# A radix search for a routing threshold on one Trainium2 core: the digit found is handed to all partitions by a matmul instead of by a transposing reduction

## The chip, the cores and the metric

One core of a Trainium2 chip runs the whole program. The metric is device time in microseconds (us), the median of three runs. Engines are named as in the profile: PE is TensorE (PEld its weight loads), DVE VectorE, ACT ScalarE, POOL GpSimd, SP the queue that issues DMAs.

## The reference

The computation is a chain of three layers. A decayed linear attention over 4 batches, 8 heads, 768 steps and head size 64 gives 3072 rows of 512. A greedy mixture of experts follows: each of 8 experts takes at most 384 tokens, in the order of the logits. A gated unit ends it.

```python
def _moe_ref(x, w_gate, w1, w2):
    cap = N // E                        # 384
    logits = x @ w_gate
    for idx in np.argsort(-logits.flatten()):
        tok, e = idx // E, idx % E
        if assigned[tok] >= 0 or counts[e] >= cap: continue
        assigned[tok] = e; counts[e] += 1
    for e in range(E):
        out[assigned == e] = np.maximum(x[assigned == e] @ w1[e], 0) @ w2[e]

def _moe2_ref(x, w_gate, w_val, w_out):
    return (sigmoid(x @ w_gate) * (x @ w_val)) @ w_out
```

## The kernel before

**Attention block (lines 268 to 663).** 24 units (4 batches, 6 chunks of 128 steps) pass through a software pipeline on all engines. `scale_k` (L454, POOL) makes the tile `ks` that PE transposes one slot later (L600). Between the second and the third `scale_k` POOL also makes the constant tables of the routing (`number_tables`, `filled_tables`), between the third and the fourth the tables derived from others (`derived_tables`); `link` lets POOL wait for each such instruction before the next.

**Routing.** Rather than sort, the kernel closes one expert at a time. One routing finds the threshold key at which some expert fills up, marks the tokens above it as assigned, numbers the members of the expert that is full, and gathers their rows. A key has 32 bits, taken as `DIGITS` = 7 digits of 5 bits, `RADIX` = 32. Per digit there were two visits of PE:

- DVE compares all keys with the 32 rungs of `ladder` (`compare`, L861, two halves into `above`); PE counts per expert and rung (L1129, 6 matmuls); DVE copies the counts (L911, `partial`);
- PE folds them (L1138, 4 matmuls into `PS_K`); DVE runs `threshold` (L871 compare with `room`, L872 maximum, giving one `flag` per partition, L873 a transposing reduction that adds the flags of each group of 32 partitions and leaves the sum on all of them, `digit_at`); then DVE makes the next key (L916, `prefix`) and compares again, and `raise_by` (L867) prepares the digit after that.

After the digits come the visits `V_TIE` (L1142 to L1144), `V_COUNT` (L1146), `V_RANK` (L1149, L1150) and `V_IDS` (L1155).

**Rounds.** The first routing stands alone, with nothing beside it. Then come 8 rounds of `one_round`. A round computes one expert and the gated unit for its 384 tokens with three matmuls per product (high and low parts, L1168 to L1170 with 384 columns, L1246 to L1248 with 512). In the first seven rounds the routing of the next expert is threaded between these matmuls. Where a visit stands on PE is set by the table `visit_at`: `step` counts the columns that PE has streamed, 2200 of them are one planned us (`us(t)`), and after each group of three matmuls the visits that are due are issued. PE runs in order and has no other way round a visit whose data isn't there. On DVE, whose queue is in order too, `route_until` puts the DVE part of a visit ahead of the next `h_low`, `h2_low` or `product` once the planned time has passed; `piece_low` (L1028) makes low parts of streamed weights, and `p_low` (L1023) the low part of the product `pf` (L1019).

In each digit of the plan, 6.8 planned us long, the counting visit stood at 0 and the folding visit at 2.2. The round loop is a hardware loop on DVE, ACT, POOL and SP for rounds 0 to 6, and unrolled on PE. In round 0 alone, POOL still makes low parts of resident weights (L262) as its `gate_done` and `val_done` come.

Of the kernel before, what the change touches and what calls it, by code (L numbers as in the profile page):

```python
# [13 lines left out]
P = 128  # L14


def retention_moe_glu_kernel(nc, q, k, v, w_router, w1, w2, w_gate, w_val, w_out, decay, out):
# [14 lines left out]
    with ctx:  # L32
        def sb(name, shape, dt):
            return ctx.enter_context(nc.sbuf_tensor(name, shape, dt))
# [17 lines left out]
        DIGITS = -(-32 // RADIX_BITS)  # L52
        NEG = -3.4028234663852886e38
        BIG = 1.0e6
        PREP_CHAIN = 13
        ROUTE_CHAIN = 78
        CHAIN_START = PREP_CHAIN
        TABLES = 7 + (TT - 1) + 6 + 3 + 3

        RING = 8  # L60
        STREAMED = KF + 2 * KD + RING
# [9 lines left out]
        V_TIE = 2 * DIGITS  # L71
        FOLD = P // RADIX
        V_COUNT = V_TIE + 1
        V_RANK = V_COUNT + 1
# [22 lines left out]
        def us(t):  # L97
            return int(t * COLUMNS_PER_US)

        DIGIT_GAP, LATE_GAP, PART_GAP = us(6.8), us(5), us(2)  # L100
        visit_at = [us(1) + vis // 2 * DIGIT_GAP + us((0, 2.2)[vis % 2]) for vis in range(2 * DIGITS)]
        visit_at += [visit_at[-1] + (n + 1) * LATE_GAP for n in range(3)]
        expert_at = visit_at[V_RANK]
        part_at = [expert_at + us(1) + n * PART_GAP for n in range(PARTS)]
# [42 lines left out]
        counted_fresh = sb("counted_fresh", [P, E], BF16)  # L147
        partial = sb("partial", [P, E, FOLD], F16)
        reached = sb("reached", [P, E], BF16)
        flag = sb("flag", [P, 1], F32)  # L150
        digit_at = sb("digit_at", [P, 1], F32)
        expert_f = sb("expert_f", [P, 1], F32)
        expert_id = sb("expert_id", [P, 1], I32)
        id_sums = sb("id_sums", [P, TT + 1], F32)
# [3 lines left out]

        segment = sb("segment", [P, E, U], BF16)
        unit_ones = sb("unit_ones", [P, U], BF16)  # L160
        ladder = sb("ladder", [P, RADIX], F32)
        raised = sb("raised", [P, U], F32)
# [5 lines left out]
        edges = sb("edges", [P, TT - 1], F32)  # L168
        below = sb("below", [P, P], BF16)
        ones = sb("ones", [P, P], BF16)  # L170
        fold = sb("fold", [P, FOLD, FOLD, RADIX], F16)
        at_above = nc.sbuf_base
        above = sb("above", [P, U, RADIX], BF16)
# [94 lines left out]
        with ExitStack() as actx:  # L268
# [113 lines left out]
            def _(pool):  # L382
# [17 lines left out]
                def number_tables():  # L400
                    count(column[:, :], [[1, P]], 0)
                    count(expert_iota[:, :], [[1, E]], 0)
                    count(priority[:, :], [[-1, E]], E)
                    count(position[:, :, 0], [[0, U]], 0, 1)
                    count(position[:, :, 1], [[P, U]], 0)
                    count(ladder[:, :], [[1, RADIX]], 1)
                    count(shift[:, :], [[-RADIX_BITS, DIGITS]], RADIX_BITS * (DIGITS - 1))

                def filled_tables():
                    for j in range(TT - 1):  # L410
                        fill(edges[:, j:j + 1], float((j + 1) * P))
                    fill(ones[:, :], 1.0)
                    fill(fold[:, :, :, :], 0.0)
                    fill(below[:, :], 1.0)
                    fill(segment[:, :, :], 1.0)
                    fill(unit_ones[:, :], 1.0)
                    fill(id_sums[:, TT:TT + 1], 0.0)
                    fill(unassigned[:, :], 1.0)
                    fill(assigned[:, :, :], 0.0)
                    fill(room[:, :], float(CAP))  # L420

                def derived_tables():
                    pool.wait_ge(tables_made, made[0])
                    link(nc.gpsimd.memset(segment[:, :, 0:1], 0.0))

                    link(pool.affine_select(out=below[:, :], in_=below[:, :], compare_op=ALU.is_gt, fill=0.0,
                                            base=0, pattern=[[1, P]], channel_multiplier=-1))
                    link(pool.affine_select(out=fold[:, :, :, :], in_=fold[:, :, :, :], compare_op=ALU.not_equal, fill=1.0,
                                            base=0, pattern=[[-RADIX, FOLD], [0, FOLD], [-1, RADIX]], channel_multiplier=1))
                    assert made[0] == TABLES, made[0]  # L430
# [400 lines left out]
        def _(dve):  # L831
# [22 lines left out]
            def flat(ap):  # L854
                return ap.rearrange("p e u -> p (e u)")

            def compare(keys):

                for half in range(2):
                    tiles = slice(half * U // 2, (half + 1) * U // 2)  # L860
                    nc.vector.tensor_tensor(above[:, tiles, :], keys[:, tiles].unsqueeze(2).to_broadcast([P, U // 2, RADIX]),  # L861
                                            ladder[:, :].unsqueeze(1).to_broadcast([P, U // 2, RADIX]),
                                            ALU.is_ge).then_inc(route_ready if half else half_compared, 1)

            def raise_by(keys, j):

                count_only(nc.vector.scalar_tensor_tensor(raised[:, :], keys, float(RADIX), digit_f[:, j, :], ALU.mult, ALU.add))  # L867
# [35 lines left out]
            def route(vis, i):  # L903

# [1 line left out]
                    return  # L906

                dve.wait_ge(route_done, i * VISITS + vis)
                if vis < V_TIE and vis % 2 == 1:

                    nc.vector.tensor_copy(partial[:, :, :], PS_R[:, 0:FOLD * E].rearrange("p (e t) -> p e t", e=E)).then_inc(route_ready, 1)  # L911
                elif vis < V_TIE:

                    j = vis // 2
                    threshold()
                    link(nc.vector.scalar_tensor_tensor(prefix[:, :], digit_at[:, :].to_broadcast([P, U]), -float(RADIX),  # L916
                                                        raised[:, :], ALU.mult, ALU.add))
                    compare(prefix)
                    if j + 1 < DIGITS:
                        raise_by(prefix[:, :], j + 1)  # L920
                elif vis == V_TIE:

                    threshold()
                    count_only(nc.vector.tensor_scalar(is_on[:, :], prefix[:, :], digit_at[:, :], None, ALU.is_equal))
                    link(nc.vector.tensor_scalar(is_above[:, :], prefix[:, :], digit_at[:, :], None, ALU.is_gt))
# [192 lines left out]
        def _(pe):  # L1118
            pe.wait_ge(tables_made, TABLES)

            def visit(vis, i):
                if vis < V_TIE and vis % 2 == 0:

                    for t in range(0, U, FOLD):
                        if t == 0:
                            pe.wait_ge(half_compared, i * DIGITS + vis // 2 + 1)
# [8 lines left out]
                if vis < V_TIE:  # L1135
# [178 lines left out]
```

## Time and profile before

| | |
|---|---|
| median of 3 runs | 1115.22 us (1115.11 to 1117.47) |
| the profiled execution | 1115.11 us, of which the span of instructions is 1113.0 us |
| PE busy | 1050.6 us, 94% of the span |
| DVE busy | 632.1 us, 57% |
| ACT busy | 344.3 us, 31% |
| POOL busy | 132.6 us, 12% |
| PE's share of the chain that ended last | 81% |

The profile shows one execution. The span runs from its first to its last instruction; the 2.1 us to the execution's own time lie around it. Matmuls are pipelined, so that a matmul's duration overlaps the next one's; what a matmul costs in a stream is read from the distance of the starts. Idle time is given ahead of a row in square brackets, with what ended it.

### The profile page before, as it was taken

How to read it: one execution, taken by the hardware profiler on the slowest of the kernel's cores; microseconds unless marked ns; L12 is line 12 of the kernel's file. 1: busy time of each engine (PE TensorE's matmuls, PEld its weight loads, DVE VectorE, ACT ScalarE, POOL GpSimd, SP SyncE). 2: the span in 40 equal slices, each digit the busy share in tenths (PEclk: the TensorE clock that was granted, in tenths of full speed). 3: DMA queues.
4: the chain of work that ended last, by engine and by line, in shares of the span. 5: the costliest groups of instructions: out<-in, count | busy, mean ns of one | idle time of the engine just before them, and what ended most of it. 6: DMA issues, size and time to landing. Idle time of an engine off the chain costs nothing.

```text
span 1113.0 us, 20477 instructions
## 1 busy us (share of the span) xinstructions
PE 1050.6 (94%) x7536; PEld 973.7 (87%) x7536; DVE 632.1 (57%) x1720; ACT 344.3 (31%) x659; POOL 132.6 (12%) x159
## 2 busy tenths in 40 slices
PE   6999922999999999999999999999999999999996
PEld 5888812989999999999999999999999999999995
DVE  3665468778366646664566456654675476634211
ACT  3444422332243224322432234223422342224210
POOL 5555301033010101000100110011001100110001
PEclk9999955999999999999999999999999999999998
DMA  9999443312041213212321222122312131214000
GB/s 205 246 243 246 111 125 104 115 39 85 20 124 58 69 37 105 77 48 57 98 83 48 58 86 95 39 67 71 110 39 67 58 115 38 67 54 118 18 1 28
DMA packets 172988, 96.69 MB, mean 87 GB/s; under 512 B 80224, under 2 KB 158048, under 8 KB 172896
## 3 DMA queue, kind: packets, MB, share of 16 engines
q1 hardware_dynamic: 169056, 82.92, 28.1%
q0 software_dynamic: 3840, 12.59, 3.8%
q8 instruction: 52, 0.85, 0.3%
q14 instruction: 40, 0.33, 0.1%
HBM read 82.90 MB, written 12.58 MB: 86 GB/s over the span
## 4 chain that ended last, share of the span: by engine, by line
PE 81%; DVE 4%; issue 1%; POOL 0%; DMA 0%; ACT 0%; DVEq 0%; POOLq 0%
PE bank L1168 21%; PE bank L1170 20%; PE bank L1169 20%; PE bank L1246 6%; PE bank L1248 6%; PE bank L1247 6%; PE bank L1163 1%; PE bank L1129 1%; DVE above L861 1%; PE bank L1138 1%; PE bank L1155 0%; DVE onehot L977 0%; DMA xg<-xrows,ids 0%; DVE ring L1028 0%; POOL out_dram L743 0%
## 5 line engine op out<-in xcount | busy, mean ns | idle before, releaser
L1168 PE MATMUL bank<-h2h,resident 128*128 128x384 f32 x768 | 260.7, 339 | 0.0
L1170 PE MATMUL bank<-h2h,resident 128*128 128x384 f32 x768 | 257.9, 336 | 0.0
L1169 PE MATMUL bank<-h2l,resident 128*128 128x384 f32 x768 | 257.4, 335 | 0.0
L1019 DVE TENSOR_TENSOR pf<-bank,gate 128x384 f32<-128x384 f32 x96 | 53.4, 556 | 167.3 <-PE bank L1170 167.1
L1169 PEld LDWEIGHTS bank<-h2l,resident 128*128 128x128 f32 x768 | 144.2, 188 | 3.4
L1168 PEld LDWEIGHTS bank<-h2h,resident 128*128 128x128 f32 x768 | 144.2, 188 | 3.5
L1170 PEld LDWEIGHTS bank<-h2h,resident 128*128 128x128 f32 x768 | 144.1, 188 | 0.0
L773 ACT ACTIVATE ring<-ring_raw 128x512 fp32r<-128x512 f32 x192 | 118.3, 624 | 64.5 <-DMA ring_raw<-in_moe_w_out_dram 41.9
L1028 DVE TENSOR_TENSOR ring<-ring_raw,ring 128x512 fp32r<-128x512 f32 x192 | 127.4, 689 | 0.0
L793 ACT ACTIVATE ph<-pf 128x384 fp32r<-128x384 f32 x96 | 50.4, 525 | 240.8 <-DVE pf L1019 240.8
L789 ACT ACTIVATE gate<-bank 128x384 f32<-128x384 f32 x96 | 47.1, 491 | 201.2 <-PE bank L1170 198.5
L1168 PE MATMUL bank<-xh,ring 128*128 128x384 f32 x256 | 89.1, 348 | 0.0
L1168 PE MATMUL bank<-hh,ring 128*128 128x384 f32 x256 | 88.7, 346 | 0.0
L1023 DVE TENSOR_TENSOR pl<-pf,ph 128x384 fp32r<-128x384 f32 x96 | 54.7, 570 | 56.8 <-ACT ph L793 56.8
L1170 PE MATMUL bank<-xh,ring 128*128 128x384 f32 x256 | 85.9, 336 | 0.0
L1169 PE MATMUL bank<-xl,ring 128*128 128x384 f32 x256 | 85.8, 335 | 0.0
L1170 PE MATMUL bank<-hh,ring 128*128 128x384 f32 x256 | 85.8, 335 | 0.0
L1169 PE MATMUL bank<-hl,ring 128*128 128x384 f32 x256 | 85.7, 335 | 0.0
L729 POOL DMA_INDIRECT xg<-xrows,ids x24 | 23.7, 986 | 499.4 <-DVE ids L993 494.5
L1246 PE MATMUL bank<-ring,ph 128*128 128x512 f32 x192 | 76.6, 399 | 0.0
L1248 PE MATMUL bank<-ring,pl 128*128 128x512 f32 x192 | 75.8, 395 | 0.0
L1247 PE MATMUL bank<-ring,ph 128*128 128x512 f32 x192 | 75.6, 394 | 0.0
(170 smaller groups left out, 1671.6 us busy)
## 6 DMA issues: line engine op xcount, KB each, us to landing
ring_raw<-in_moe_w_dram SPq DMA_DIRECT2D x128, 256.0 KB, 3.0
ring_raw<-in_moe_w_out_dram SPq DMA_DIRECT2D x64, 256.0 KB, 2.9
qraw<-in_q_dram SPq DMA_DIRECT2D x24, 256.0 KB, 4.5
kraw<-in_k_dram SPq DMA_DIRECT2D x24, 256.0 KB, 5.1
vraw<-in_v_dram SPq DMA_DIRECT2D x24, 256.0 KB, 5.2
xrows<-xrow SPq DMA_DIRECT2D x24, 256.0 KB, 4.0
resident_raw<-in_moe_w_gate_dram SPq DMA_DIRECT2D x12, 256.0 KB, 4.5
resident_raw<-in_moe_w_val_dram SPq DMA_DIRECT2D x12, 256.0 KB, 4.7
```

Source lines behind the costliest of these rows:

```text
L773: nc.scalar.activation(ring[:, n % RING, 0, :], ring_raw[n % RING][:, :], ACT.Copy).then_inc(piece_hi, 1)
L789: nc.scalar.activation(gate[:, f % 2, :], bank[2 * (f % 2)][:, 0:CAP], ACT.Sigmoid).then_inc(gate_ready, 1)
L793: nc.scalar.activation(ph[:, f % 2, :], pf[:, f % 2, :], ACT.Copy).then_inc(ph_ready, 1)
L1019: nc.vector.tensor_tensor(pf[:, f % 2, :], bank[2 * (f % 2) + 1][:, 0:CAP], gate[:, f % 2, :], ALU.mult).then_inc(p_ready, 1)
L1023: nc.vector.tensor_tensor(pl[:, f % 2, :], pf[:, f % 2, :], ph[:, f % 2, :].bitcast(F32), ALU.subtract).then_inc(pl_ready, 1)
L1028: nc.vector.tensor_tensor(ring[:, s, 1, :], ring_raw[s][:, :], ring[:, s, 0, :].bitcast(F32), ALU.subtract).then_inc(piece_lo, 1)
L1168: nc.tensor.matmul(ps, wh, xhi, start=start, stop=False)
L1169: nc.tensor.matmul(ps, wh, xlo, start=False, stop=False)
L1170: return nc.tensor.matmul(ps, wl, xhi, start=False, stop=stop)
L1246: nc.tensor.matmul(PS_OUT[j][:, :], ph[:, f % 2, toks], wh, start=f == 0, stop=False)
L1247: nc.tensor.matmul(PS_OUT[j][:, :], ph[:, f % 2, toks], wl, start=False, stop=False)
L1248: last = nc.tensor.matmul(PS_OUT[j][:, :], pl[:, f % 2, toks], wh, start=False, stop=f == KG - 1)
```

## The change

Per digit there are now three visits. DVE stops after the maximum (`flag`, now bf16) and signals PE. PE multiplies the flags of all 128 partitions by a constant matrix `weighted_ones[:, j, :]`, whose entries are 32^-j / 4; the sum, times that weight, stands in `PS_K[:, 0:1]` on every partition. DVE reads it from there as a per-partition scalar. The digits are weighted in advance (`digit_f` times 32^-j) and each digit has its own ladder, so that keys need no raising; `raise_by` goes. The added tables are made by POOL: `weight` and `weighted_ones` in `filled_tables`, six ladders in `derived_tables`. The plan keeps 6.8 planned us per digit, with visits at 0, 1.7 and 4; the visits after the digits follow 1.8 planned us later than before.

```diff
-        visit_at = [us(1) + vis // 2 * DIGIT_GAP + us((0, 2.2)[vis % 2]) for vis in range(2 * DIGITS)]
+        visit_at = [us(1) + vis // 3 * DIGIT_GAP + us((0, 1.7, 4)[vis % 3]) for vis in range(3 * DIGITS)]
...
-        flag = sb("flag", [P, 1], F32)
-        digit_at = sb("digit_at", [P, 1], F32)
+        flag = sb("flag", [P, 1], BF16)
...
                 def filled_tables():
+                    for j in range(DIGITS):
+                        fill(weight[:, j:j + 1], float(RADIX) ** -j)
+                        fill(weighted_ones[:, j, :], float(RADIX) ** -j / FOLD)
...
                 def derived_tables():
                     pool.wait_ge(tables_made, made[0])
+                    for j in range(1, DIGITS):
+                        link(nc.gpsimd.tensor_scalar(ladder[:, j, :], ladder[:, 0, :], float(RADIX) ** -j, None, ALU.mult))
...
-            def threshold():
-
-                link(nc.vector.tensor_tensor(reached[:, :], PS_K[:, 0:E], room[:, :], ALU.is_ge))
-                link(nc.vector.reduce_max(flag[:, :], reached[:, :], AX_X))
-                link(nc.vector.tensor_reduce(digit_at[:, :], flag[:, :].to_broadcast([P, RADIX]), axis=AX_X, op=ALU.add,
-                                             apply_transpose=True))
...
-                link(nc.vector.tensor_scalar(digit_f[:, :, :], digit_i[:, :, :], 1.0, None, ALU.add))
-                compare(digit_f[:, 0, :])
-                raise_by(digit_f[:, 0, :], 1)
+                link(nc.vector.scalar_tensor_tensor(digit_f[:, :, :], digit_i[:, :, :], 1.0,
+                                                    weight[:, :].unsqueeze(2).to_broadcast([P, DIGITS, U]), ALU.add, ALU.mult))
+                compare(0, digit_f[:, 0, :])
...
+                elif vis < V_TIE and vis % 3 == 2:
+
+                    link(nc.vector.tensor_tensor(reached[:, :], PS_K[:, 0:E], room[:, :], ALU.is_ge))
+                    nc.vector.reduce_max(flag[:, :], reached[:, :], AX_X).then_inc(route_ready, 1)
                 elif vis < V_TIE:
 
-                    j = vis // 2
-                    threshold()
-                    link(nc.vector.scalar_tensor_tensor(prefix[:, :], digit_at[:, :].to_broadcast([P, U]), -float(RADIX),
-                                                        raised[:, :], ALU.mult, ALU.add))
-                    compare(prefix)
-                    if j + 1 < DIGITS:
-                        raise_by(prefix[:, :], j + 1)
+                    j = vis // 3
+                    link(nc.vector.scalar_tensor_tensor(prefix[:, :], digit_f[:, 0, :] if j == 1 else prefix[:, :], PS_K[:, 0:1],
+                                                        digit_f[:, j, :], ALU.subtract, ALU.add))
+                    compare(j, prefix)
...
+                elif vis < V_TIE:
+
+                    last = nc.tensor.matmul(PS_K[:, 0:1], weighted_ones[:, vis // 3, :], flag[:, :], start=True, stop=True)
```

On PE, in a round, four groups of three matmuls behind the folding visit of a digit (`hh` and `ring` are the operands of the expert's second product), before:

```order
L1169 MATMUL bank<-hl,ring 128x384
L1170 MATMUL bank<-hh,ring 128x384
L1168 MATMUL bank<-hh,ring 128x384
L1169 MATMUL bank<-hl,ring 128x384
L1170 MATMUL bank<-hh,ring 128x384
```

The same place in the changed kernel, whose lines are numbered 3 lower here:

```order
L1166 MATMUL bank<-hl,ring 128x384
L1167 MATMUL bank<-hh,ring 128x384
L1136 MATMUL bank<-flag,weighted_ones 128x1
L1165 MATMUL bank<-hh,ring 128x384
L1166 MATMUL bank<-hl,ring 128x384
```

One matmul with one moving column is added between two groups, once per digit.

On DVE, in a round, at the start of the gated unit (`pf` and `pl` belong to its first tile; `ring_raw_82` and `ring_raw_83` are streamed pieces), before:

```order
L838 REGISTER_ALU
L916 SCALAR_TENSOR_TENSOR prefix<-digit_at,raised 128x24
L838 REGISTER_ALU
L861 TENSOR_TENSOR above<-prefix,ladder 128x384 x2
L1019 TENSOR_TENSOR pf<-bank,gate 128x384
L1023 TENSOR_TENSOR pl<-pf,ph 128x384
L1027 REGISTER_ALU
L1028 TENSOR_TENSOR ring<-ring_raw_82,ring 128x512
L1027 REGISTER_ALU
L1028 TENSOR_TENSOR ring<-ring_raw_83,ring 128x512
L908 REGISTER_ALU
L911 CAST partial<-bank 128x32
```

And in the changed kernel:

```order
L1013 TENSOR_TENSOR pf<-bank,gate 128x384
L1017 TENSOR_TENSOR pl<-pf,ph 128x384
L1021 REGISTER_ALU
L1022 TENSOR_TENSOR ring<-ring_raw_82,ring 128x512
L1021 REGISTER_ALU
L1022 TENSOR_TENSOR ring<-ring_raw_83,ring 128x512
L902 REGISTER_ALU
L913 SCALAR_TENSOR_TENSOR prefix<-prefix,bank,digit_f 128x24
L843 REGISTER_ALU
L866 TENSOR_TENSOR above<-prefix,ladder 128x384 x2
L902 REGISTER_ALU
L905 CAST partial<-bank 128x32
```

The last comparison of the routing moves from ahead of the product `pf` to behind both pieces.

On POOL, in the attention block, from the last filled tables to the fourth `scale_k`, before:

```order
L398 MEMSET room 128x8
L454 TENSOR_TENSOR ks<-kraw,dec 128x512
L424 MEMSET segment 128x8
L426 AFFINE_SELECT below<-below 128x128
L428 AFFINE_SELECT fold<-fold 128x512
L454 TENSOR_TENSOR ks<-kraw,dec 128x512 x4
```

And in the changed kernel:

```order
L398 MEMSET room 128x8
L459 TENSOR_TENSOR ks<-kraw,dec 128x512
L428 TENSOR_SCALAR ladder<-ladder 128x32 x6
L429 MEMSET segment 128x8
L431 AFFINE_SELECT below<-below 128x128
L433 AFFINE_SELECT fold<-fold 128x512
L459 TENSOR_TENSOR ks<-kraw,dec 128x512 x4
```

Six instructions, each waited for, come ahead of the fourth `ks`. Fourteen `MEMSET` rows, seven of 128x1 and seven of 128x128, come ahead of the third.

## Rows read from the trace of the kernel before

**Rows 1.** Busy time (us, share, instructions), and granted clock in 40 slices
```profile
PE 1050.6 (94%) x7536; PEld 973.7 (87%) x7536; DVE 632.1 (57%) x1720; ACT 344.3 (31%) x659; POOL 132.6 (12%) x159
...
PEclk9999955999999999999999999999999999999998
```

**Rows 2.** PE's waits, 195 to 1113: for whom, us in total, times, longest
```profile
PE bank L1142 <- DVE tied_before L932: 1.1, 1, 1.1
```

**Rows 3.** Timeline of PE around L1146: start, duration, line, shapes
```profile
365.39 0.33 PE L1169 MATMUL bank<-h2l,resident 128*128 128x384 f32 x1
365.57 0.34 PE L1170 MATMUL bank<-h2h,resident 128*128 128x384 f32 x1
365.75 0.18 PE L1146 MATMUL bank<-counted_fresh,ones 128*128 128x8 bf16 x1
365.79 0.48 PE L1246 MATMUL bank<-ring,ph 128*128 128x512 f32 x1
366.10 0.39 PE L1247 MATMUL bank<-ring,ph 128*128 128x512 f32 x1
366.33 0.40 PE L1248 MATMUL bank<-ring,pl 128*128 128x512 f32 x1
```

**Rows 4.** Timeline of PE around a counting visit of six matmuls
```profile
345.09 0.34 PE L1170 MATMUL bank<-h2h,resident 128*128 128x384 f32 x1
345.27 0.32 PE L1129 MATMUL bank<-choice,above 128*128 128x32 bf16 x6
345.43 0.42 PE L1168 MATMUL bank<-h2h,resident 128*128 128x384 f32 x1
345.69 0.33 PE L1169 MATMUL bank<-h2l,resident 128*128 128x384 f32 x1
```

**Rows 5.** Timeline of POOL, 2 to 19
```profile
2.28 1.20 POOL L444 TENSOR_SCALAR_AFFINE_SELECT pick<-pick 128x8 f32<-128x8 f32 x4
...
13.36 0.20 POOL L398 MEMSET ones<- 128x128 bf16 x1
13.50 0.52 POOL L398 MEMSET fold<- 128x512 f16 x1
...
14.37 0.09 POOL L398 MEMSET id_sums<- 128x1 f32 x1
14.40 0.11 POOL L398 MEMSET unassigned<- 128x24 f32 x1
...
18.30 1.48 POOL L454 TENSOR_TENSOR ks<-kraw,dec 128x512 f32<-128x512 f32 x1 [0.81 <-DMA vraw<-in_v_dram]
```

**Rows 6.** Timeline of PE, 16 to 20
```profile
16.23 0.66 PE L600 MATMUL bank<-ident,ks 128*128 128x128 f32 x4 [0.20 <-POOL ks L454]
...
19.89 0.61 PE L600 MATMUL bank<-ident,ks 128*128 128x128 f32 x4
```

**Rows 7.** PE's busy time in stretches: us, PE busy first, granted clock
```profile
17.00:30.00 13.00, 13.00 (x218) 11.80 (x216) 7.10 (x14) 5.80 (x12) 5.07 (x4) 1.00 1.22 245
30.00:60.00 30.00, 29.70 (x447) 26.19 (x446) 19.66 (x33) 13.52 (x29) 15.32 (x14) 1.00 1.01 241
60.00:90.00 30.00, 30.00 (x459) 26.77 (x455) 18.78 (x35) 13.08 (x28) 15.37 (x15) 1.00 1.05 243
```

**Rows 8.** Timeline of one digit of the first routing, and of L1144
```profile
150.60 0.16 DVE L872 TENSOR_REDUCE flag<-reached 128x1 f32<-128x8 bf16 x1
150.79 0.21 DVE L873 TRANSPOSE_TENSOR_REDUCE digit_at<-flag 128x1 f32<-128x32 f32 x1
151.04 0.18 DVE L916 SCALAR_TENSOR_TENSOR prefix<-digit_at,raised 128x24 f32<-128x24 f32 x1
151.26 1.03 DVE L861 TENSOR_TENSOR above<-prefix,ladder 128x384 bf16<-128x384 f32 x2
...
170.46 0.21 PE L1144 MATMUL bank<-counted,ones 128*128 128x8 bf16 x1
170.71 0.16 DVE L935 TENSOR_TENSOR limit<-room,bank 128x8 f32<-128x8 f32 x1 [0.60 <-PE bank L1144]
```

**Rows 9.** Timeline of DVE at the start of round 1
```profile
307.50 1.88 DVE L1034 COPY orow<-bank 128x512 f32<-128x512 f32 x3
311.22 0.19 DVE L911 CAST partial<-bank 128x32 f16<-128x32 f32 x1 [1.84 <-issue]
```

**Rows 10.** Timeline of DVE in round 1, from the first product
```profile
350.25 0.55 DVE L1019 TENSOR_TENSOR pf<-bank,gate 128x384 f32<-128x384 f32 x1
351.39 0.56 DVE L1023 TENSOR_TENSOR pl<-pf,ph 128x384 fp32r<-128x384 f32 x1 [0.59 <-ACT ph L793]
351.87 1.29 DVE L1028 TENSOR_TENSOR ring<-ring_raw,ring 128x512 fp32r<-128x512 f32 x2
353.07 0.18 DVE L911 CAST partial<-bank 128x32 f16<-128x32 f32 x1
```

**Rows 11.** Timeline of DVE and POOL in round 0
```profile
236.64 2.38 DVE L1028 TENSOR_TENSOR ring<-ring_raw,ring 128x512 fp32r<-128x512 f32 x2
...
237.08 1.39 POOL L262 TENSOR_TENSOR resident<-resident_raw,resident 128x512 fp32r<-128x512 f32 x1 [0.79 <-PE bank L1170]
```

More of the change, by code:

```diff
@@ L54, in retention_moe_glu_kernel @@
         BIG = 1.0e6
-        PREP_CHAIN = 13
-        ROUTE_CHAIN = 78
+        PREP_CHAIN = 12
+        ROUTE_CHAIN = 58
         CHAIN_START = PREP_CHAIN
-        TABLES = 7 + (TT - 1) + 6 + 3 + 3
+        TABLES = 7 + 3 * DIGITS - 1 + (TT - 1) + 6 + 3 + 3
         RING = 8
@@ L69, in retention_moe_glu_kernel @@
         assert KF == RING and 2 * KD == RING and OUT_STREAMED <= KG and TT == 3 and LATE % LATE_EACH == 0
-        V_TIE = 2 * DIGITS
+        V_TIE = 3 * DIGITS
         FOLD = P // RADIX
@@ L160, in retention_moe_glu_kernel @@
         unit_ones = sb("unit_ones", [P, U], BF16)
-        ladder = sb("ladder", [P, RADIX], F32)
-        raised = sb("raised", [P, U], F32)
+        ladder = sb("ladder", [P, DIGITS, RADIX], F32)
+        weight = sb("weight", [P, DIGITS], F32)
         shift = sb("shift", [P, DIGITS], I32)
@@ L170, in retention_moe_glu_kernel @@
         ones = sb("ones", [P, P], BF16)
+        weighted_ones = sb("weighted_ones", [P, DIGITS, P], BF16)
         fold = sb("fold", [P, FOLD, FOLD, RADIX], F16)
@@ L405, in number_tables @@
                     count(position[:, :, 1], [[P, U]], 0)
-                    count(ladder[:, :], [[1, RADIX]], 1)
+                    count(ladder[:, 0, :], [[1, RADIX]], 1)
                     count(shift[:, :], [[-RADIX_BITS, DIGITS]], RADIX_BITS * (DIGITS - 1))
                 def filled_tables():
+                    for j in range(DIGITS):
+                        fill(weight[:, j:j + 1], float(RADIX) ** -j)
+                        fill(weighted_ones[:, j, :], float(RADIX) ** -j / FOLD)
                     for j in range(TT - 1):
@@ L855, in flat, with compare @@
                 return ap.rearrange("p e u -> p (e u)")
-            def compare(keys):
+            def compare(j, keys):
                 for half in range(2):
@@ L861, in compare @@
                     nc.vector.tensor_tensor(above[:, tiles, :], keys[:, tiles].unsqueeze(2).to_broadcast([P, U // 2, RADIX]),
-                                            ladder[:, :].unsqueeze(1).to_broadcast([P, U // 2, RADIX]),
+                                            ladder[:, j, :].unsqueeze(1).to_broadcast([P, U // 2, RADIX]),
                                             ALU.is_ge).then_inc(route_ready if half else half_compared, 1)
-            def raise_by(keys, j):
-                count_only(nc.vector.scalar_tensor_tensor(raised[:, :], keys, float(RADIX), digit_f[:, j, :], ALU.mult, ALU.add))
-            def threshold():
-                link(nc.vector.tensor_tensor(reached[:, :], PS_K[:, 0:E], room[:, :], ALU.is_ge))
-                link(nc.vector.reduce_max(flag[:, :], reached[:, :], AX_X))
-                link(nc.vector.tensor_reduce(digit_at[:, :], flag[:, :].to_broadcast([P, RADIX]), axis=AX_X, op=ALU.add,
-                                             apply_transpose=True))
             def prepare():
@@ L908, in route @@
                 dve.wait_ge(route_done, i * VISITS + vis)
-                if vis < V_TIE and vis % 2 == 1:
+                if vis < V_TIE and vis % 3 == 1:
                     nc.vector.tensor_copy(partial[:, :, :], PS_R[:, 0:FOLD * E].rearrange("p (e t) -> p e t", e=E)).then_inc(route_ready, 1)
+                elif vis < V_TIE and vis % 3 == 2:
+                    link(nc.vector.tensor_tensor(reached[:, :], PS_K[:, 0:E], room[:, :], ALU.is_ge))
+                    nc.vector.reduce_max(flag[:, :], reached[:, :], AX_X).then_inc(route_ready, 1)
                 elif vis < V_TIE:
-                    j = vis // 2
-                    threshold()
-                    link(nc.vector.scalar_tensor_tensor(prefix[:, :], digit_at[:, :].to_broadcast([P, U]), -float(RADIX),
-                                                        raised[:, :], ALU.mult, ALU.add))
-                    compare(prefix)
-                    if j + 1 < DIGITS:
-                        raise_by(prefix[:, :], j + 1)
+                    j = vis // 3
+                    link(nc.vector.scalar_tensor_tensor(prefix[:, :], digit_f[:, 0, :] if j == 1 else prefix[:, :], PS_K[:, 0:1],
+                                                        digit_f[:, j, :], ALU.subtract, ALU.add))
+                    compare(j, prefix)
                 elif vis == V_TIE:
-                    threshold()
-                    count_only(nc.vector.tensor_scalar(is_on[:, :], prefix[:, :], digit_at[:, :], None, ALU.is_equal))
-                    link(nc.vector.tensor_scalar(is_above[:, :], prefix[:, :], digit_at[:, :], None, ALU.is_gt))
+                    count_only(nc.vector.tensor_scalar(is_on[:, :], prefix[:, :], PS_K[:, 0:1], None, ALU.is_equal))
+                    link(nc.vector.tensor_scalar(is_above[:, :], prefix[:, :], PS_K[:, 0:1], None, ALU.is_gt))
                     link(nc.vector.tensor_tensor(tied[:, :, :], choice[:, :, :], per_token(is_on[:, :]), ALU.mult))
@@ L1121, in visit @@
             def visit(vis, i):
-                if vis < V_TIE and vis % 2 == 0:
+                if vis < V_TIE and vis % 3 == 0:
                     for t in range(0, U, FOLD):
                         if t == 0:
-                            pe.wait_ge(half_compared, i * DIGITS + vis // 2 + 1)
+                            pe.wait_ge(half_compared, i * DIGITS + vis // 3 + 1)
                         if t == U // 2:
@@ L1134, in visit @@
                     pe.wait_ge(route_ready, i * (VISITS - 1) + vis + 1)
-                if vis < V_TIE:
+                if vis < V_TIE and vis % 3 == 1:
                     for t in range(FOLD):
```

## The prediction

> **What bounds the kernel now.** I read the busy times first: PE has 94% of the span, the next engine 57% [rows 1]. Then PE's waits in the rounds, from 195 on: in 918 us PE waits once, 1.1 us, for DVE at a `V_TIE` visit; that is in round 0 [rows 2]. So in the rounds PE is the bound, and what DVE needs for a digit costs nothing as long as it is ready when PE comes. A change there is worth what it adds to PE's stream, and whatever wait it makes. Then the stretches of the attention block: PE is busy without a gap from 17 on, at the full granted clock of 2.4 GHz [rows 7]; there too a delay of PE is never made good. Only the first routing, about 145 to 183, is a chain of DVE and PE with nothing beside it, in the slices whose granted clock is 0.5, that is 1.2 GHz [rows 1].
>
> **The rounds: 49 more visits.** Seven rounds with a routing, seven digits each, one more matmul. No row shows a matmul of one column, but L1146 is a visit of one matmul with 8 columns and the same kind of stationary matrix. Undisturbed matmuls of 384 columns start 0.17 to 0.18 apart (365.39, 365.57) and those of 512 columns 0.23 apart (366.10, 366.33) [rows 3]. From 365.57 to 366.10 would then be 0.18 for L1170 and 0.23 for L1246, 0.41; it is 0.53. The visit costs 0.12. A counting visit of six matmuls: from 345.09 to 345.69 is 0.60, of which two matmuls of 384 would take 0.35, so 0.25 [rows 4]. Between one and six matmuls the cost rises by 0.13, about 0.026 a matmul, and 0.10 stands for the visit as such: PE stops for the semaphore and can't load weights ahead. I take 0.13 for each new visit, since nearly all stand between matmuls of 384 columns: 49 x 0.13 = 6.4. Bounds: 0.026, if only the step per matmul were paid, gives 1.3; 0.15 gives 7.4.
>
> The Trainium skill ("TensorE: Matmul & The Clock Gate", section "Wait — 56ns, not 53.3ns?") says that start to start never drops below about 25 ns, however few columns a matmul has. The 0.026 per matmul inside a visit agrees with it. Taken as the whole price of one more small matmul it would make an estimate of 49 x 0.025 = 1.2; the 0.12 of the lone visit speaks against that.
>
> **New waits of PE in the rounds.** I went through a round of the plan, placing each visit at its group of three matmuls (0.52 a group) and each DVE part behind what stands ahead of it. Four places are near.
>
> - *The first fold of a round.* At the loop's turn DVE idles 1.84 after the rows' copies and makes `partial` at 311.22 to 311.41 [rows 9]. The fold was due five groups behind the counting visit (3.2 planned us), now four (2.7): with the count at 309.04, four groups 2.08 and 0.25 for the visit, at 311.37. From `partial`'s end to a matmul's start there are some 0.06, so PE waits 0.1, in six rounds 0.6. In round 0 DVE comes to it late by its eight pieces; I count 0.3 more. Together 0.9, bounds 0 and 2.
> - *The last counting visit.* Its comparison now stands behind `pf`, `pl` and two pieces, where it stood ahead of them. I count from the start of the counting visit before it, which is at 345.27 [rows 4]. PE: 0.25 for that visit, four groups, 0.2 for the fold, four groups, 0.13 for the new visit, five groups: 13 x 0.52 + 0.58 = 7.3. DVE: the gated unit's first tile ends one group behind the fold, and the product can start at 3.3, as it no longer waits for the comparison; `pl` starts 1.14 later, the pieces 0.48 after that, and `prefix`, where `partial` stood, 1.20 later, at 6.1 [rows 10]. With 0.28 for `prefix` and 1.03 for both halves the first is ready at 6.95, the second at 7.43. PE comes at 7.3, and 0.1 later wants the second: the first is in time, the second some 0.07 late with its signal: 7 x 0.07 = 0.5. Bounds 0, and 7 if the slip is 1 in each round.
> - *The same in round 0.* There a DVE operation that comes while POOL works on resident weights starts only as POOL ends: two pieces took 2.38 instead of 1.29 beside L262 [rows 10, 11]. In the new order the second piece meets POOL's instruction before that one, and the comparison comes about 1.0 to 1.4 late. I take 1.0, bounds 0 and 1.5.
> - *`V_TIE` in round 0.* Between the last fold and this visit, 5.0 planned us, DVE had a product, a piece, the threshold and the visit's own work to do, and came 1.1 late [rows 2]. Now product, piece and threshold lie ahead of the new visit, and only the visit's own work lies in the 5.0 behind it. The wait goes: -1.1. Bounds -1.1 and 0.
>
> The Trainium skill ("SBUF — State Buffer", section "SBUF: two separate sides") says that a DVE instruction with two SBUF inputs contends with a GpSimd instruction that reads SBUF, and that the loser blocks for the whole instruction. The trace agrees: 1.09 more for two pieces beside one of 1.39. By it the round-0 wait is a full one rather than shared.
>
> All other DVE parts are ready 0.2 to 1.8 before PE comes; the nearest is the fourth digit's `partial`, behind `h2l` and two pieces, 0.2 early. Later visits move 1.8 planned us back; `ids` are wanted only 30 us later.
>
> **The tables.** POOL makes 14 more fills ahead of the third `ks`. A fill of 128x128 bf16 takes 0.14 (13.36 to 13.50), one of 128x1 0.03 (14.37 to 14.40) [rows 5]: 7 x 0.17 = 1.2. PE already waits for this `ks`, 0.20 at 16.23 [rows 6], so nothing covers it: 1.2 on the path. Then six linked multiplications come ahead of the fourth `ks`. Nearest rows: the linked `pick`, four in 1.20, so 0.3 each, 1.8 in all [rows 5]. Of 1.2 + 1.8 = 3.0, POOL's idle 0.81 at 18.30 is cover; that `ks` starts at 20.5 and ends, 1.48 later, at 22.0. PE wants it at 19.89 + 1.2 = 21.1 [rows 6]: 0.9 more. Sum 2.1. PE makes none of it good up to the end of the block [rows 7]. Bounds: 1.2 if the multiplications are hidden, 3.0 if each takes 0.45; 0 only if a later wait took it up, and there is none.
>
> **The first routing.** From `flag` to `prefix` lie 0.44 now (150.60, 151.04), with L873 between [rows 8]. New: `flag` 0.16, some 0.06 to PE, a matmul to the instruction behind it 0.25, as L1144 to L935 (170.46, 170.71): 0.47. So 0.03 for each of 7 digits, 0.2. `prefix` now takes a scalar per partition from PSUM; no row has that form, I take 0.06 more, 6 x 0.06 = 0.4. The L867 that goes stood in the shadow of PE's counting. `digit_f` with a second input: 0.1. Sum 0.7. Bounds: -0.7 (0.1 less per digit) and 1.8 (0.25 more).
>
> **Sum.** 6.4 + 0.9 + 0.5 + 1.0 - 1.1 + 2.1 + 0.7 = 10.5. The profiled execution took 1115.11 with a span of 1113.0; 1115.1 + 10.5 = 1125.6. That execution is 0.1 from the median of 1115.22. I forecast 1125.5.
>
> **Rivals.**
>
> - *Lone matmuls are cheap.* A one-column matmul may cost PE only the 0.026 of a further matmul in a visit: 1.3 instead of 6.4, so 10.5 - 5.1 = 5.4, 1120.5. For it: within a visit the price is that low [rows 3, 4]. Against it: L1146 is alone as well, and costs 0.12. 8%.
> - *A wait in each round.* If `prefix` and both halves come 1 us later at the last counting visit, or `partial` of the fourth digit does at its fold, each round pays a wait of 0.8: 7 x 0.8 = 5.6 more, 1131. For it: 0.2 and less of slack at both. Against: in round 1 the pieces take 1.29, in the regular step [rows 10]. 12%.
> - *The tables are hidden*, by a faster POOL or a later wait: 8.4, 1123.5. It lies in the main case's range; 10% of its own.
> - *Faster.* PE's chain per digit is shorter by a transposing reduction and L867 on DVE. If the new visits fell into PE's own shadow and the tables too, `V_TIE` would give 1.1 and the first routing 0.7: 1115.1 - 1.8 = 1113.3. What decides is the visit's price: up to 1.8 / 49 = 0.04 each it is no slower. Against: PE has no idle time in the rounds that could hold a visit [rows 2]. 3%.
>
> The forecast has the remaining 67%. Its own range is 1123.5 to 1128. Down to the cheap matmuls and up to part of the waits, the range for 8 in 10 is 1121 to 1130. About 0.2%, 2.2 us, is what can be told from no change; the last rival's 3% lie mostly within that: faster by more than it 1%, within it 3%, slower 96%.
>
> **What would show it.** PE's row of the new matmul with 56 in the profile, 49 of them in the rounds, each adding 0.12 to 0.14 between its neighbours' starts; a round in PE's repeated rows longer by 1.0 to 1.1; POOL named as what PE waits for at the third and fourth `ks`, about 1.4 and 0.9; the first routing's digit 0.1 longer; no `V_TIE` wait. Wrong it would be if PE waited more than 0.5 for DVE in each round, if the new visit cost under 0.05, or if the attention block ended at the same time as before.

## The result, and the profile after

The changed kernel takes 1127.53 us (median of 4 runs, 1126.45 to 1129.05), the kernel before, run beside it, 1115.54. The ratio is 1.0105, with a 95% interval from 1.0092 to 1.0118: it is slower, by about 12 us. The profiled execution took 1127.42 with a span of 1125.7. The forecast was 1125.5 with 1121 to 1130.

The busy times of the page, which answer to [rows 1]:

```profile
PE 1061.6 (94%) x7592; PEld 974.9 (87%) x7592; DVE 614.2 (55%) x1615; ACT 345.2 (31%) x659; POOL 133.7 (12%) x179
```

DVE has 105 instructions and 18 us less, and it buys nothing: PE has 56 instructions and 11 us more, still 94% of the span. To see where the time went, I cut the span at PE's transposes of the gathered rows, since each round begins with twelve of them. The view of that tile on PE gives the first and the last start; the kernel before, and then the one after:

```profile
L1163 PE MATMUL bank<-ident,xg x96: 272/273/475, 189.5 to 992.4; 128*128 128x128 f32 x96
```
```profile
L1160 PE MATMUL bank<-ident,xg x96: 270/272/474, 192.1 to 1005.0; 128*128 128x128 f32 x96
```

The first start is 2.6 later, the last one 12.6 later; behind it nothing changes. Read with each round's first transpose from PE's timeline, the 12.7 of the span are:

| part | before | after | more | forecast |
|---|---|---|---|---|
| start to the first routing | 144.82 | 146.83 | 2.0 | 2.1 |
| first routing, gather | 44.73 | 45.29 | 0.6 | 0.7 |
| round 0 | 115.03 | 119.19 | 4.2 | 1.2 |
| rounds 1 to 6 together | 6 x 114.44 | 692.54 | 5.9 | 6.5 |
| last part | 121.8 | 121.8 | 0.0 | 0 |

(Forecast by part: in round 0, seven lone matmuls 0.9, fold 0.3, last count 0.1, the same beside POOL 1.0, `V_TIE` -1.1; in the six others 5.5, 0.6 and 0.4.)

**The new visit.** PE's timeline around one of the new matmuls, as in [rows 3]:

```profile
349.69 0.33 PE L1166 MATMUL bank<-hl,ring 128*128 128x384 f32 x1
349.86 0.34 PE L1167 MATMUL bank<-hh,ring 128*128 128x384 f32 x1
350.04 0.18 PE L1136 MATMUL bank<-flag,weighted_ones 128*128 128x1 bf16 x1
350.08 0.42 PE L1165 MATMUL bank<-hh,ring 128*128 128x384 f32 x1
350.34 0.34 PE L1166 MATMUL bank<-hl,ring 128*128 128x384 f32 x1
```

From 349.86 to 350.34 is 0.48; two matmuls of 384 columns would take 0.35. The visit costs 0.13, though its own row is followed by the next start after only 0.04. The loss shows in the next two starts (0.04 + 0.26), so it can be read only over several rows. Over all 49 such visits the mean is 0.132.

**Round 0.** PE's waits from 195 on, which answer to [rows 2]:

```profile
PE bank L1123 <- DVE above L866: 1.8, 2, 1.3
```

The wait at `V_TIE` is gone, and two at the last counting visit have come. DVE, POOL and PE there, from their three timelines:

```profile
239.81 1.26 DVE L913 SCALAR_TENSOR_TENSOR prefix<-prefix,bank,digit_f 128x24 f32<-128x24 f32 x1
241.11 2.09 DVE L866 TENSOR_TENSOR above<-prefix,ladder 128x384 bf16<-128x384 f32 x2
```
```profile
239.19 1.85 POOL L262 TENSOR_TENSOR resident<-resident_raw,resident 128x512 fp32r<-128x512 f32 x1 [0.92 <-PE bank L1167]
241.27 1.52 POOL L262 TENSOR_TENSOR resident<-resident_raw,resident 128x512 fp32r<-128x512 f32 x1 [0.23 <-PE bank L1167]
```
```profile
241.72 0.24 PE L1123 MATMUL bank<-choice,above 128*128 128x32 bf16 x3 [0.54 <-DVE above L866]
243.26 0.24 PE L1123 MATMUL bank<-choice,above 128*128 128x32 bf16 x3 [1.30 <-DVE above L866]
...
245.07 0.63 PE L1243 MATMUL bank<-ring,ph 128*128 128x512 f32 x1
245.50 0.63 PE L1244 MATMUL bank<-ring,ph 128*128 128x512 f32 x1
```

`prefix`, undisturbed 0.24 to 0.25, lasts 1.26 and ends with POOL's first operation (239.19 + 1.85 = 241.04, against 241.07). The first half of `above` starts ahead of POOL's second operation and keeps its 0.56; the second half lasts 1.62 where e6 below has 0.55, and ends at 243.20, 0.41 behind that operation (241.27 + 1.52 = 242.79). PE waits 0.54 and 1.30. Then a thing that the forecast did not have: matmuls of 512 columns start 0.43 apart instead of 0.23 [rows 3]. PE's busy time in stretches of one execution, granted clock behind it, says why:

```profile
236.00:240.00 4.00, 4.00 (x28) 1.00 0.00 0
240.00:244.00 4.00, 2.17 (x16) 1.00 0.00 0
244.00:248.00 4.00, 4.00 (x17) 0.57 0.00 0
```

PE stood 1.8 of 4 us, and in the 4 us behind that the clock was 0.57 on average (2.4 GHz to start with, then 1.2, then 2.4 again): 4 x 0.43 = 1.7 us lost. The page's 40 slices show nothing of it.

**The tables.** POOL's timeline, as in [rows 5], and PE's, as in [rows 6]:

```profile
13.31 0.09 POOL L398 MEMSET weight<- 128x1 f32 x1
13.35 0.19 POOL L398 MEMSET weighted_ones<- 128x128 bf16 x1
...
14.54 0.12 POOL L398 MEMSET edges<- 128x1 f32 x2
...
15.96 1.04 POOL L459 TENSOR_TENSOR ks<-kraw,dec 128x512 f32<-128x512 f32 x1
17.08 2.58 POOL L428 TENSOR_SCALAR ladder<-ladder 128x32 f32<-128x32 f32 x6
...
21.18 2.49 POOL L459 TENSOR_TENSOR ks<-kraw,dec 128x512 f32<-128x512 f32 x2
```
```profile
17.05 0.66 PE L605 MATMUL bank<-ident,ks 128*128 128x128 f32 x4 [0.64 <-POOL ks L459]
...
22.28 0.66 PE L605 MATMUL bank<-ident,ks 128*128 128x128 f32 x4 [1.41 <-POOL ks L459]
```

The fourteen fills take 1.23. The six multiplications take 2.58, 0.43 each, where 0.3 was assumed. PE takes up the fourth `ks` at 22.28, 2.4 later than the 19.89 of before. At the end of the block 2.0 of the 2.4 are left.

**The first routing**, DVE's and PE's timelines of a digit, as in [rows 8]:

```profile
152.69 0.16 DVE L909 TENSOR_REDUCE flag<-reached 128x1 bf16<-128x8 bf16 x1
153.13 0.25 DVE L913 SCALAR_TENSOR_TENSOR prefix<-digit_f,bank 128x24 f32<-128x24 f32 x1 [0.28 <-PE bank L1136]
153.41 1.03 DVE L866 TENSOR_TENSOR above<-prefix,ladder 128x384 bf16<-128x384 f32 x2
```
```profile
152.91 0.18 PE L1136 MATMUL bank<-flag,weighted_ones 128*128 128x1 bf16 x1 [0.46 <-DVE flag L909]
```

From `flag` to `prefix` it is 0.44, as before: the way over PE costs what the transposing reduction did. `prefix` takes 0.25 instead of 0.18, and that is the difference, 0.07 a digit.

### The profile page after: what moved, and what is told of

The parts are those of the page before. It is cut to its first block, busy times and chain, and to the rows that moved or that the text cites. A ratio compares the mean times of both kernels' runs of the same rounds, so it can differ in the third digit from the quotient of the medians.

```text
span 1125.7 us, 20462 instructions
## 1 busy us (share of the span) xinstructions
PE 1061.6 (94%) x7592; PEld 974.9 (87%) x7592; DVE 614.2 (55%) x1615; ACT 345.2 (31%) x659; POOL 133.7 (12%) x179
## 4 chain that ended last, share of the span: by engine, by line
PE 82%; DVE 3%; issue 1%; POOL 0%; DMA 0%; ACT 0%; DVEq 0%; POOLq 0%
PE bank L1165 21%; PE bank L1167 20%; PE bank L1166 20%; PE bank L1243 6%; PE bank L1245 6%; PE bank L1244 6%; PE bank L1160 1%; PE bank L1123 1%; DVE above L866 1%; PE bank L1132 1%; PE bank L1152 0%; DVE onehot L971 0%; DMA xg<-xrows,ids 0%; DVE prefix L913 0%; POOL out_dram L748 0%
## 5 line engine op out<-in xcount | busy, mean ns | idle before, releaser
L1017 DVE TENSOR_TENSOR pl<-pf,ph 128x384 fp32r<-128x384 f32 x96 | 53.7, 560 | 52.9 <-ACT ph L798 52.7
```

Source lines behind the costliest of these rows:

```text
L1017: nc.vector.tensor_tensor(pl[:, f % 2, :], pf[:, f % 2, :], ph[:, f % 2, :].bitcast(F32), ALU.subtract).then_inc(pl_ready, 1)
```

## The experiments

**What does one more small matmul cost PE, and why?** The forecast had put 0.10 of the 0.13 down to PE's stop for the semaphore. The rival was the matmul's position alone between large ones. The kernel before gets 49 matmuls of one column, seven in a round, once without a wait, once with one on a semaphore long since raised, and once ahead of the fold's four.

```
e1   + if into is not None and lone[0] < DIGITS and us(5.5) + lone[0] * DIGIT_GAP <= at[0]:
     +     nc.tensor.matmul(into[:, 400:401], ones[:, :], unit_ones[:, 0:1], start=False, stop=False)
     +     lone[0] += 1
e2   +     pe.wait_ge(tables_made, TABLES)          (ahead of the matmul)
e3   + if i > 0:                                    (in visit, ahead of the fold's loop)
     +     nc.tensor.matmul(PS_K[:, 200:201], ones[:, :], unit_ones[:, 0:1], start=True, stop=True)
```

> The kernel before, with one more matmul of one moving column, with no consumer and no wait of its own, between two groups of three matmuls, once per digit in each of seven rounds: 49 in all. Theory A (a small matmul alone between large ones costs PE 0.13, because the next large weight load has nothing to hide behind): a round is 7 x 0.13 = 0.9 longer, the whole 6.4 us. Theory B (what costs is the stop for the semaphore, 0.10 of the 0.13): without a wait each costs 0.03, a round is 0.2 longer, the whole 1.3 us.

> The same 49 matmuls at the same places, each behind a wait for a semaphore that was reached long before. Both theories expect 6.4 us, 0.9 a round; if this is dearer than the kernel without the waits, the difference is the wait's.

> The same 49 matmuls, each put at the head of the folding visit of its digit, so that visit has five small matmuls instead of four. Both theories expect the step per matmul inside a visit, 0.026 each: 1.3 us in all, 0.2 a round. If it is 6 us instead, a small matmul costs 0.13 wherever it stands.

Measured beside a before of 1116.61: e1 1122.83 (ratio 1.0055, 1.0039 to 1.0072), e2 1123.29 (1.0056, 1.0039 to 1.0073), e3 1119.49 (1.0024, 1.0014 to 1.0033). A round of 114.44 became 115.38 in both e1 and e2 (0.94, 0.134 for each matmul) and 114.79 in e3 (0.35, 0.050 each, where both theories had 0.2). PE's timeline in e1, then in e3:

```profile
330.53 0.34 PE L1170 MATMUL bank<-hh,ring 128*128 128x384 f32 x1
330.71 0.18 PE L1180 MATMUL bank<-unit_ones,ones 128*128 128x1 bf16 x1
330.75 0.42 PE L1168 MATMUL bank<-hh,ring 128*128 128x384 f32 x1
331.01 0.34 PE L1169 MATMUL bank<-hl,ring 128*128 128x384 f32 x1
```
```profile
335.59 0.34 PE L1172 MATMUL bank<-hh,ring 128*128 128x384 f32 x1
335.77 0.18 PE L1137 MATMUL bank<-unit_ones,ones 128*128 128x1 bf16 x1
335.81 0.24 PE L1140 MATMUL bank<-partial,fold 128*128 128x8 f16 x4
335.91 0.42 PE L1170 MATMUL bank<-hh,ring 128*128 128x384 f32 x1
336.17 0.34 PE L1171 MATMUL bank<-hl,ring 128*128 128x384 f32 x1
```

The starts around e1's matmul, which waits for nothing, are those of the changed kernel's visit to 0.01. So the semaphore is not the cause, and this sentence of the forecast falls; its price stands. What costs is that a small matmul stands by itself: in company it costs 0.05, twice the forecast's 0.026 for a further one. That the hidden part is the loading of the next large matmul's weights fits the late second start (0.26), but no run took that load away.

**Round 0.** The fall of the clock was expected to go if PE did not stand. Two edits of the changed kernel bring this about in different ways: e5 has the one-column matmul ahead of the last counting visit 1.0 planned us earlier (38.0 instead of 39.0), so that DVE's `prefix` comes before its pieces; e6 takes POOL's operations out of DVE's way.

```
e5   + visit_at[17] = us(38.0)
e6   - pool.wait_ge(val_done if k % 2 else gate_done, k // 2 + 1)
     + pool.wait_ge(val_done if k % 2 else gate_done, k // 2 + 3)
```

> The changed kernel with one number of the plan changed: the last digit-making matmul in a round stands at 38.0 planned us instead of 39.0, so that DVE's last comparison goes between the product and its low part, ahead of the two pieces. Theory W (in round 0 the comparison queues behind pieces that meet POOL's work, PE waits 1.8 for it, and the pause lets the clock fall to 1.2 GHz for some 3.5 us): both go in round 0, 1.8 + 1.7 = 3.5 us less, so 1124.0; the other rounds keep their length within 0.1. Rival: the clock falls for another reason; then only 1.8 us go.

> The changed kernel with POOL's twelve low parts of resident weights in round 0 waiting for tiles two further on, so that none of them is beside the last comparison; the plan is untouched. If POOL's instruction is what makes the comparison late (theory W), PE waits under 0.1 at the last counting visit in round 0 too, as in the other rounds, and 3.5 us go. If the order on DVE alone makes it late, the 1.8 stay.

Measured beside a before of 1116.4: e5 1124.07 (1.0067, 1.005 to 1.0083), e6 1124.27 (1.0068, 1.0051 to 1.0085). Round 0 fell from 119.19 to 115.28 and 115.37, and the stretches of PE in e6 have no low clock any more:

```profile
236.00:240.00 4.00, 4.00 (x28) 1.00 0.00 0
240.00:244.00 4.00, 4.00 (x29) 1.00 0.00 0
244.00:248.00 4.00, 4.00 (x25) 1.00 0.02 4
```

DVE's timeline in e6, at the place where `prefix` took 1.26 and `above` 2.09:

```profile
239.87 0.24 DVE L913 SCALAR_TENSOR_TENSOR prefix<-prefix,bank,digit_f 128x24 f32<-128x24 f32 x1
240.14 1.02 DVE L866 TENSOR_TENSOR above<-prefix,ladder 128x384 bf16<-128x384 f32 x2
```

Both remove 3.8 to 3.9, more than the waits of 1.84, and 1.84 + 1.7 = 3.5 of it are the waits and the clock. So PE's standing comes from DVE's operations beside POOL's. The Trainium skill ("SBUF — State Buffer", section "SBUF: two separate sides"), named in the forecast for the full wait, was borne out: `prefix` ended 0.03 behind POOL's operation, and the half of `above` that met the next one ended only behind it too.

The low clock is less sure than the waits. No execution without the two waits has it. With them, it came again when the changed kernel was profiled once more (e10): round 0 118.78, clock 0.50 from 243.7 to 247.1. But in e4, the changed kernel with later tables (below), PE waited the same twice and the clock stayed:

```profile
242.24 0.24 PE L1123 MATMUL bank<-choice,above 128*128 128x32 bf16 x3 [0.54 <-DVE above L866]
243.77 0.24 PE L1123 MATMUL bank<-choice,above 128*128 128x32 bf16 x3 [1.30 <-DVE above L866]
```
```profile
244.00:248.00 4.00, 4.00 (x25) 1.00 0.00 0
```

Its round 0 took 117.85, 1.3 less than the 119.19. So the waits can bring the clock down, in two of three executions here, but they do not always.

The same edit on the kernel before tests the fourth point, that its wait at `V_TIE` is of that kind:

> The kernel before with one edit: in the expert's rounds POOL takes each multiplication two gate blocks (two products) later than before (the wait for val_done or gate_done counts two more). This takes POOL's 1.39 to 1.85 us operations away from the DVE's compare of the last digit in round 0, where the kernel before has PE's wait for V_TIE (1.08 us). Theory M (the pauses of round 0 come from DVE's compare beside POOL's operations): the wait of about 1.1 us at the end of round 0 goes, its 115.0 becomes 113.9 to 114.2, rounds 1 to 6 stay at 114.4, in all -1.1 us or ratio 0.999. Theory W (the wait comes from the number of columns between the last digit's visits, so POOL's place doesn't matter): no change, round 0 stays within 0.3 of 115.0. Rival against both: with POOL's buffers two products later a product is ready later for the down matmuls and each round gains a wait: over 0.3 us in every round, in all above +2.

Measured: 1115.49 beside 1116.38, ratio 0.9992 (0.9983 to 1.0001), PE waits for nobody from 195 on, rounds 1 to 6 unchanged. DVE's timeline shows the first comparison behind the last digit as short as it should be, where the kernel before has 1.11 beside POOL's operation at 241.68:

```profile
242.09 0.24 DVE L924 TENSOR_SCALAR is_on<-prefix,digit_at 128x24 f32<-128x24 f32 x1
```

The wait of 1.08 is gone, but round 0 of the profiled execution fell only from 115.03 to 114.78. That is over the 113.9 to 114.2 of theory M and within the 0.3 that theory W allowed. It is the wait itself, gone with the plan untouched, that speaks for M. In this execution the low clock at the round's start lasted from 190.05 to 195.2, in that of before from 189.55 to 192.5. That is 2.2 us longer at half the clock, so 1.1 lost: by these rows the gain is there, and a later rise of the clock covers it; why the rise comes later was not tested. By the interval e8 is not shown to be faster than the kernel before.

**The tables.** e4 moves the three steps that make them to a later batch; e7 has this and e5's edit.

```
e4   - if b == 0 and c == 1:      (number_tables, filled_tables)
     + if b == 1 and c == 4:
     - if b == 0 and c == 2:      (derived_tables)
     + if b == 1 and c == 5:
```

> The changed kernel with all constant tables of the routing made by POOL later: between the scale_k of the second batch's fifth and sixth chunk, and behind it, instead of between the second and fourth of the first batch. Theory T (the added table instructions hold up the third and fourth ks and so PE): PE's waits for ks go, the attention block ends 2.0 us earlier than in the changed kernel, the whole is 2.0 us (1.8 to 2.3) shorter than the changed kernel's 1127.5: 1125.4. Rival: the attention block is bound by its loads; then nothing changes.

> The changed kernel with later tables and the earlier last digit together. If the shares add up: 2.0 + 3.5 less than the changed kernel, 1122.0. What is left over the kernel before, 6.8 us, would be 49 x 0.13 = 6.4 for the lone matmuls, 0.5 for the first routing, 0.6 or less for the first folds, less 1.1 for the V_TIE wait and 0.2 for the old wait for ks.

Measured beside 1116.4: e4 1126.74 (1.0088, 1.0071 to 1.0104), e7 1124.05 (1.0063, 1.0046 to 1.008). Both expectations missed: e4 was to take 1125.4 and e7 1122.0, and e7 is no faster than e5, which has its earlier digit alone (1124.07). The first routing did not start earlier: 146.97 in e4, 147.73 in e7, against 146.83. PE's waits in e4, 14 to 147:

```profile
PE bank L621 <- DVE logits L538: 2.6, 4, 0.7
...
PE bank L598 <- DVE qs L545: 0.4, 1, 0.4
```
```profile
35.26 1.50 DVE L545 TENSOR_TENSOR qs<-qraw,dec 128x512 f32<-128x512 f32 x1 [3.25 <-DMA vraw<-in_v_dram]
```

The 2.0 for `ks` are gone, 1.3 more for `logits` and 0.4 for `qs` have come. PE's transposes of `ks`, one group for each unit, show where. The fourth starts at 20.27, 2.0 ahead of the changed kernel, and the sixth (31.25) keeps that. At the eighth (43.53 against 44.30) 0.8 is left: the `qs` of DVE's row above had waited 3.25 for the load `vraw`, where the changed kernel has 0.49. By the fourteenth (76.05 against 75.90) nothing is left. The first loss, 1.3, is not the moved tables': e2, with the tables of before, has it at the same place (43.34 against the 42.03 of before), behind a `qs` that waited 3.48 for `vraw`. That fits the rival in e4's expectation, a block bound by its loads. The second, 0.7 between 69.8 and 76.1, is in e4 and e7 only; what makes it was not tested. This left the cause of the 2.0 open: was it the tables, or do such blocks differ anyhow? So the kernel before got the added tables alone, in the change's place and read by nothing (fourteen fills and six multiplications; the expectation below counts them as sixteen and seven), and the changed kernel was profiled again.

```
e9   + fill(weight[:, j:j + 1], float(RADIX) ** -j)
     + fill(weighted_ones[:, j, :], float(RADIX) ** -j / FOLD)
     + link(nc.gpsimd.tensor_scalar(added[:, j, :], ladder[:, :], float(RADIX) ** -j, None, ALU.mult))
```

> The kernel before, with only the change's added table work in its place: eight more pairs of memsets (the weights and the weighted ones) and seven more multiplications of the ladder, none of them read by anything; the routing is the one before. It leaves out nothing. Theory T (the added table work makes POOL's ks late, and PE's waits for it move the end of the attention block): PE waits for ks about 2.0 us around 17 to 22 us, the routing starts at 146.8 or later, against 144.8 to 146.0 in the kernels whose tables are those of before; in all +2.0, ratio 1.0018. Theory S (the block's end varies by over 1 us between executions, and what PE loses at 17 to 22 us it gets back in the waits behind): PE waits for ks the same 2.0 us, but the routing starts at 145 to 146 and the whole is within 0.8 of before. In both all rounds stay at 114.4 and round 0 at 115.0.

> The changed kernel once more, unedited, for how far its parts repeat from one execution to the next. Theory T: the routing starts at 146.8 within 0.3 again. Theory S: it starts anywhere from 145.8 to 147.8. The lone matmuls: rounds 2 to 6 at 115.4 within 0.1. Round 0: 119.2 if the fall of the clock behind the two waits for DVE (0.54 and 1.30 us) comes each time; 117.5 if it came once by chance. In all ratio 1.0105 as before, or 1.009 without the fall.

Measured beside 1116.38: e9 1118.42 (1.0015, 1.0006 to 1.0024), e10 1128.48 (1.0109, 1.0093 to 1.0124). PE's timeline in e9:

```profile
17.41 1.06 PE L608 MATMUL bank<-ident,ks 128*128 128x128 f32 x4 [0.23 <-POOL ks L462]
22.53 0.66 PE L608 MATMUL bank<-ident,ks 128*128 128x128 f32 x4 [0.89 <-POOL ks L462]
```

PE waits 1.1 for `ks`, where both theories had 2.0, but it takes up the fourth at 22.53, where the changed kernel has 22.28. The routing of e9, which is the one before, starts at 147.07. The whole is 2.0 longer, with an interval of 0.7 to 2.7, as theory T had it. Over the profiled executions, e4 and e7 apart, the routing starts at 144.82, 144.93, 145.86, 146.01 and 145.26 with the tables of before (mean 145.4), and at 146.83, 146.73, 147.11, 147.18 and 147.07 with the added ones in the change's place (mean 147.0). The groups don't overlap. The tables cost 1.6 on average of the profiles; the 2.0 of one pair holds some 0.4 of what differs between executions of one kernel. In e10 the rounds did not repeat within the expected 0.1: three of the rounds 1 to 6 took 115.67 to 115.70. PE's rows place it at the first fold, which starts 2.35 behind its counting visit where PE runs through, and 2.65 in these three.

## Why the prediction was right

It was right in sign and size, and most terms in their mechanism. By the profiles the changed kernel is 12.7 longer where 10.5 were forecast. Round 0 was forecast 3.0 too low, the other parts together 0.8 too high, so part of the closeness is luck.

- *Lone matmuls, 6.4 forecast.* 49 x 0.132 = 6.5. Read off L1146, one row of another kind of visit, the price held to 0.01. The reason given with it (the stop for the semaphore) was wrong, as e1 and e2 show. The rival that they are cheap fell.
- *First fold of a round and last counting visit, 0.6 and 0.4 in rounds 1 to 6.* The rounds rose by 5.9, of which 42 x 0.132 = 5.5 are the lone matmuls. 0.4 are left for both, where 1.0 was forecast. The first fold, 2.35 behind its counting visit where PE runs through, comes 0 to 0.13 late, 0.25 in the six rounds together; at the last counting visit PE's rows show no wait, only 0.02 more to the matmul behind it. In e10 the first folds lose 1.0 in all. So the first term was of the right kind and differs between executions, and the last counting visit's, 0.4, was not there. In four of the six rounds of the first profile the whole rise is 0.93 to 0.95, no more than the lone matmuls alone make in e1. The rival with a wait in each round fell with it.
- *Round 0.* The step that failed is "the same in round 0", 1.0 with bounds 0 and 1.5. The mechanism was right (DVE's comparison behind POOL's operations, once for `prefix` and once for the second half of `above`), but it was counted once, and only as a delay. It measured 1.84 of waiting and 1.7 of low clock behind it, 3.5 in all; in e4 the waiting alone came. `V_TIE` gave back its 1.1 as forecast. 0.9 more came from a low clock at the round's start that lasted 4.6 us instead of 2.9 (PE starts at 192.1, full clock at 196.8). Round 0 is then 0.9 - 1.1 + 1.8 + 1.7 + 0.9 = 4.2, as measured. The 0.9 differs between executions: in e10 the low stretch was 3.2.
- *Tables, 2.1.* 2.0 in the pair of profiles, 1.6 over ten executions. Two errors cancelled in part: each multiplication took 0.43, not 0.3, and the fourth `ks` 1.04, not 1.48. PE took it up 2.4 later, and 0.4 of that was gone by the end of the block, though the forecast had no later wait that could take any of it up. It had read three stretches up to 90 as free of gaps; but PE waits 0.2 for `logits` at 52.9 in the kernel before and not in the changed one, and in e2 and e4 it waits for a `qs` whose load came late.
- *First routing, 0.7.* 0.6. The 0.06 for a scalar from PSUM was 0.07; the 0.03 for the way over PE was 0.

What is not settled: why PE loses 0.7 around 70 to 76 us when the tables are in the later batch, why the load `vraw` comes late in some executions, what decides whether the clock falls behind the two waits, and what part of a lone matmul's 0.13 is the next weight load.

## What to carry over

Where one engine is busy for 94% of the span, taking two instructions from another engine's chain by giving this one a small instruction was a loss each time: 0.13 per lone matmul, 0.05 where it was joined to a visit that is there anyway. I would price an added matmul by the starts of the large ones around it, not by its own row. A wait of PE in a full stream is to be priced with the low clock that can follow it, and a table that is filled once is not free if the engine that fills it feeds the bound one at that moment.

## What the runs showed of the hardware

- The granted clock fell to 1.2 GHz in a stream that had been busy at 2.4 GHz for 44 us, after PE stood 0.54 and 1.30 us with three small matmuls between; 3.4 us later it was at 2.4 again. The fall cost about as much as the waits (1.7 and 1.84). It came in two profiled executions with these waits and not in a third (e4). The single wait of 1.08 in the kernel before and in e9 was followed by no such fall.
- A one-column matmul between matmuls of 384 columns costs 0.13 with or without a semaphore wait, 0.05 directly ahead of four other small ones.
- DVE's 128x24 `prefix` took 1.26 beside a POOL operation, 0.24 without it; half an `above` 1.62, and 0.55 without it. A linked POOL multiplication of 128x32 took 0.41 to 0.43, while a 128x1 fill started 0.03 to 0.04 ahead of the next instruction.
- Executions of kernels that are alike up to there differ in parts that the total hides: the attention block's end by 1.2 us (144.82 to 146.01 with the tables of before), the low stretch of clock at round 0's start by 2.3 us (2.9 in before and e5, 5.2 in e8 and e4), PE's first fold of a round by 0.3 us.
